# Experts with one token tile and the third token tile: the up product with tokens stationary and weights moving; attention scores in 64x64 array tiles; the last wait on SyncE

## What is computed

```python
# attention, per batch and head
y[t] = r[t] @ (state + outer(u * k[t], v[t]))
state = w[:, None] * state + outer(k[t], v[t])
# dense network, 384 -> 2048 -> 384
h = x @ w_in;  g = maximum(h, 0) + alpha * minimum(h, 0);  x = g @ w_out
# experts, 384 -> 1024 -> 384, at most 384 rows each, in order of the rows
e = argmax(x @ w_gate);  p = softmax(x @ w_gate)[e]
out[i] = p * (maximum(disp[e] @ w1[e], 0) @ w2[e])[pos[i]]   # 0 for rows over capacity
```

## Time and profile before

| | |
|---|---|
| median of 3 runs | 455.86 us (455.79 to 456.08) |
| the profiled execution | 453.51 us |
| its span, first to last instruction | 451.8 us |
| PE busy | 425.0 us (94%) |
| DVE, ACT, POOL busy | 257.5, 197.8, 175.9 us |
| granted clock of PE over the span | 0.981 |
| expert stage | 291.8 to 443.0 us |

### The profile page before, as it was taken

The page is one execution under the profiler, slowest core; times in us unless marked ns, Lnnn a source line. Parts: engine busy times, 40 slices in busy tenths (PEclk is TensorE's granted clock), DMA queues, the critical chain, the costliest instruction groups (busy, mean ns, idle before and its releaser), DMA issues.

```text
span 451.8 us, 8997 instructions
## 1 busy us (share of the span) xinstructions
PE 425.0 (94%) x3141; PEld 410.1 (91%) x3141; DVE 257.5 (57%) x555; ACT 197.8 (44%) x450; POOL 175.9 (39%) x189
## 2 busy tenths in 40 slices
PE   6799999999999999999999986899999999998892
PEld 5688889999999999999999985699999999998891
DVE  6688876766435343543437563444659574658730
ACT  2689944341311113111323332334668575558640
POOL 4999525554323523244435861511120210012102
PEclk9899999999999999999999997999999999999996
DMA  7996024437950100000012440684676875563000
GB/s 253 399 326 200 3 83 154 154 100 261 371 201 0 54 1 0 0 28 24 0 35 81 142 145 17 215 316 123 206 237 184 245 209 176 161 209 89 11 19 7
DMA packets 33935, 61.43 MB, mean 136 GB/s; under 512 B 4655, under 2 KB 26911, under 8 KB 33889
## 3 DMA queue, kind: packets, MB, share of 16 engines
q1 hardware_dynamic: 31008, 55.53, 37.7%
q0 software_dynamic: 2880, 5.29, 3.5%
HBM read 47.53 MB, written 14.79 MB: 138 GB/s over the span
## 4 chain that ended last, share of the span: by engine, by line
PE 80%; DVE 7%; ACT 5%; issue 3%; POOL 2%; DMA 0%; POOLq 0%; ACTq 0%; DVEq 0%
PE bank L1146 20%; PE bank L1161 19%; PE bank L1271 16%; PE bank L1300 14%; ACT scores L610 2%; PE bank L1052 2%; PE bank L1079 2%; PE bank L1115 2%; ACT w_high L595 1%; PE bank L1107 1%; PE bank L1258 1%; PE bank L1067 1%; DVE neg L883 1%; DVE act_full L889 1%; DVE xe_low L1002 1%
## 5 line engine op out<-in xcount | busy, mean ns | idle before, releaser
L509 POOL TENSOR_TENSOR g_low<-act_full,g_high 128x384 fp32r<-128x384 f32 x63 | 63.7, 1010 | 115.2 <-ACT g_high L641 115.2
L641 ACT ACTIVATE g_high<-act_full 128x384 fp32r<-128x384 f32 x64 | 33.7, 526 | 150.0 <-DVE act_full L889 137.4
L1146 PE MATMUL bank<-x_split,w_high 128*128 (+1 forms) x384 | 98.4, 337 | 0.0
L883 DVE TENSOR_SCALAR neg<-bank,alpha_sb 128x384 f32<-128x384 f32 x64 | 39.2, 613 | 71.6 <-PE bank L1146 71.5
L565 POOL DMA_INDIRECT out<-y_out,token x24 | 24.8, 1032 | 125.2 <-ACT y_out L728 124.3
L1146 PEld LDWEIGHTS bank<-x_split,w_high 128*128 128x128 f32 x384 | 69.0, 188 | 0.2 <-issue 0.2
L1161 PE MATMUL bank<-w_high,g_high 128*128 128x384 f32 x189 | 65.1, 344 | 1.2 <-POOL g_low L509 1.2
L1146 PE MATMUL bank<-x_split,w_low 128*128 (+1 forms) x192 | 64.4, 336 | 0.0
L1161 PE MATMUL bank<-w_high,g_low 128*128 128x384 f32 x189 | 63.8, 338 | 0.0
L1161 PE MATMUL bank<-w_low,g_high 128*128 128x384 f32 x189 | 63.8, 337 | 0.0
L1271 PE MATMUL bank<-xe_high,w_high 128*128 128x256 f32 (+1 forms) x192 | 58.0, 302 | 1.7 <-DVE xe_low L1002 1.7
(11 more groups left out here) (127 smaller groups left out, 800.7 us busy)
## 6 DMA issues: line engine op xcount, KB each, us to landing
w_raw<-chunks SPq DMA_DIRECT2D x96, 192.0 KB, 3.2
w_raw<-chunks SPq DMA_DIRECT2D x32, 384.0 KB, 3.1
rk_in<-att_rk SPq DMA_DIRECT2D x12, 704.0 KB, 6.5
routed_rows<-fill SPq DMA_DIRECT2D x1, 5211.0 KB, 17.7
xe<-routed_rows SPq DMA_DIRECT2D x7, 579.0 KB, 5.3
v_in<-att_v SPq DMA_DIRECT2D x12, 200.0 KB, 5.2
out<-fill SPq DMA_DIRECT2D x1, 2304.0 KB, 22.9
x_split<-x_split POOLq DMA_DIRECT2D x18, 48.0 KB, 2.5
```

Source lines behind the costliest of these rows:

```text
L509: pool.tensor_tensor(gl[:, f % 4, :], act_full[:, f % 2, :], gh[:, f % 4, :].bitcast(f32), ALU.subtract).then_inc(s_gl, 1)
L641: act.activation(gh[:, f % 4, :], act_full[:, f % 2, :], ACT.Copy).then_inc(s_gh, 1)
L883: dve.tensor_scalar(neg[:, f % 2, :], h, 0.0, alpha_sb[:, f:f + 1], ALU.min, ALU.mult)\
L1146: last = mm(bank[f % 4][:, 0:G], a[:, f, w], x[:, kc, bass.ds(g * G, G)], start=kc == 0 and i == 0, stop=kc == KC - 1 and i == 2)
```

## The change

1. **One-tile experts** (`rows < P + 1`): the up product is turned round. `flip_up` holds a 128x128 block of tokens stationary and moves the w1 of four chunks, 512 columns, so 9 matmuls make half of the hidden layer, in a bank, with tokens on the partitions. DVE takes the relu into `gn` (`flip_relu`), PE transposes it in eight 128x128 pieces (`flip_turn`), ACT and DVE make the high and low parts (`flip_high`, `flip_low`), and `expert_down` goes on as before. The next expert's tokens are turned between the halves.
2. **Three-tile experts**: tiles 0 and 1 as before with 256 columns, the third by the same flipped way, its transposes in the middle of the first down product. The down products go 1, 2, 0 and so do the copies and scatters (`Y_ORDER`).
3. ACT's `flip_high(e, 2)` and DVE's `flip_relu(e, 2, ..)` and `flip_low(e, 2, ..)` run for every expert, also where there is no third tile; PE raises their semaphores (`s_fh[1]` before the down products, `s_ft[1]` after the first of two, or after five of eight chunks where there is one). PE's next use of banks 0 to 3 waits for them (`flip_banks_free`).
4. The low part of w1 (`split_low1`) moves from DVE to POOL, ahead of the expert's scatters.
5. **Scores** in four array tiles: two matmuls of 64 stationary columns in place of one of 128.
6. ACT in attention: diagonals, kn copy, y copy, with the y copy of the same step; kn copies wait for ruk, ruk no longer for kn copies, `k_turn` for both.
7. SP takes over the wait for the last scatter.

```diff
             sp.wait_ge(s_out, 16 * GT * (E - 1))
+            sp.wait_ge(s_last, 16 * GT)
...
-            for e in range(1, E):
-                for i in reversed(range(GT)):
-                    y_scatter(e - 1, i)
-
-                pool.wait_ge(s_out, e * 16 * GT)
-                pool.sem_inc(s_gone, 1)
-            for i in reversed(range(GT)):
-                y_scatter(E - 1, i, s_last)
-
-            pool.wait_ge(s_last, GT * 16)
+            def split_low1(e, f):
...
+            for e in range(E):
+                if e + FIRST < E:
+                    for f in range(NFE):
+                        split_low1(e + FIRST, f)
+                for i in Y_ORDER:
+                    y_scatter(e, i, s_out if e < E - 1 else s_last)
+                if e < E - 1:
+                    pool.wait_ge(s_out, (e + 1) * 16 * GT)
+                    pool.sem_inc(s_gone, 1)
...
             def kn_copy(t):
                 act.wait_ge(s_kt, t + 1)
+                if t:
+                    act.wait_ge(s_ruk, t + 1)
...
             for t in range(T):
-                if t:
-                    x_high(t - 1)
+                if t + 1 < T:
+                    diagonals(t + 1)
                 if t + 2 < T:
                     kn_copy(t + 2)
-                if t + 1 < T:
-                    diagonals(t + 1)
+                x_high(t)
                 if CT <= t < CT + EARLY:
                     split_high(t - CT)
-            x_high(T - 1)
...
+            def flip_high(e, i):
+                act.wait_ge(s_step, e * NFE + FFN_STEPS)
+                for half in range(2):
+                    act.wait_ge(s_ft[i // 2], 2 * e + half + 1)
+                    act.activation(egh[:, half * HF:(half + 1) * HF, i * P:(i + 1) * P],
+                                   bank[2 + half][:, :].rearrange("p (f n) -> p f n", f=HF), ACT.Copy)\
+                       .then_inc(s_fc[i // 2], 1)
+            for e in range(E):
+                with act.If(rows[e] < P + 1):
+                    if e < E - 1:
+                        for i in range(GT):
+                            xe_high(e + 1, i, bank[4 + GT - 1 - i])
+                    flip_high(e, 0)
                     if FIRST <= e + 1 < E:
-                        split_high2(e + 1, f)
-
-            for e in range(E):
-                with act.If(rows[e] < 2 * P + 1):
-                    ups(e, 2 * P)
+                        for f in range(NFE):
+                            split_high2(e + 1, f)
+                    act.sem_inc(s_mgh, NFE)
...
+                flip_high(e, 2)
                 for f in range(NFE):
                     if e + FIRST < E:
                         split_high1(e + FIRST, f)
                     if f in (3, 5, 7):
-                        y_copy(e, (7 - f) // 2)
+                        y_copy(e, Y_ORDER[(f - 3) // 2])
...
-                dve.wait_ge(s_kn, t + 1)
+                if t < 2:
+                    dve.wait_ge(s_kn, t + 1)
+                dve.wait_ge(s_kt, t + 1)
...
+            def flip_relu(e, i, half):
+                dve.wait_ge(s_fh[i // 2], 2 * e + half + 1)
+                if i:
+                    dve.wait_ge(s_ft[0], 2 * e + 2)
+                elif e:
+                    dve.wait_ge(s_ft[1], 2 * e)
+                dve.tensor_scalar(gn[:, half * HF * P:(half + 1) * HF * P], bank[half][:, :], 0.0, None, ALU.max)\
+                   .then_inc(s_fr[i // 2], 1)
+            def flip_low(e, i, half):
+                dve.wait_ge(s_fc[i // 2], 2 * e + half + 1)
...
+                if i:
+                    op.then_inc(s_fl, 1)
+                else:
+                    op.then_inc(s_mgl, HF)
+            for e in range(E):
+                with dve.If(rows[e] < P + 1):
+                    flip_relu(e, 0, 0)
+                    if e < E - 1:
+                        for i in range(GT):
+                            xe_low(e + 1, i, bank[4 + GT - 1 - i])
+                    flip_relu(e, 0, 1)
+                    for half in range(2):
+                        flip_low(e, 0, half)
                     if FIRST <= e + 1 < E:
-                        split_low2(e + 1, f)
-
-            for e in range(E):
-                with dve.If(rows[e] < 2 * P + 1):
-                    ups(e, 2 * P)
+                        for f in range(NFE):
+                            split_low2(e + 1, f)
...
+                for half in range(2):
+                    flip_relu(e, 2, half)
+                for half in range(2):
+                    flip_low(e, 2, half)
                 if e < E - 1:
                     keep_meta(e + 1)
-                if e + FIRST < E:
-                    for f in range(NFE):
-                        split_low1(e + FIRST, f)
...
+                reuse(pe, s_kn, t)
...
-                    for h2 in range(2):
-                        p = slice(h2 * HALF, (h2 + 1) * HALF)
-                        last = mm(a_bank(t, h2)[:, a * P:(a + 1) * P], k_hat[p, t % 3, a, :],
-                                  r_hat[p, t % RH, a, :], start=True, stop=True)
+                    for half in range(2):
+                        for h2 in range(2):
+                            p = slice(h2 * HALF, (h2 + 1) * HALF)
+                            tokens = slice(half * HALF, (half + 1) * HALF)
+                            last = mm(a_bank(t, h2)[tokens, a * P:(a + 1) * P], k_hat[p, t % 3, a, tokens],
+                                      r_hat[p, t % RH, a, :], start=True, stop=True)
...
+            def flip_banks_free(e, b):
+                if b < 2:
+                    pe.wait_ge(s_fr[1], 2 * (e - 1) + 1 + b)
+                else:
+                    pe.wait_ge(s_fl, 2 * (e - 1) + b - 1)
...
+            def flip_up(e, i, half):
+                slot = e * NFE % SLOTS + half * HF
+                w1_ready(pe, e, half * HF + HF - 1)
                 if i:
-                    last.then_inc(s_yd[i], 1)
+                    pe.wait_ge(s_mgl, e * NFE + HF + half + 1 + C_MGL)
+                elif e:
+                    pe.wait_ge(s_mgl, (e - 1) * NFE + HF + half + 1 + C_MGL)
+                    flip_banks_free(e, half)
+                for kc in range(KC):
+                    for m, (x, w) in enumerate(((xeh, wh), (xeh, wl), (xel, wh))):
+                        last = mm(bank[half][:, :].rearrange("p (f n) -> p f n", f=HF),
+                                  x[:, e % 2, kc, i * P:(i + 1) * P], w[:, slot:slot + HF, kc * P:(kc + 1) * P],
+                                  start=kc == 0 and m == 0, stop=kc == KC - 1 and m == 2)
+                last.then_inc(s_fh[i // 2], 1)
+            def flip_turn(e, i):
+                for half in range(2):
+                    pe.wait_ge(s_fr[i // 2], 2 * e + half + 1)
+                    if i:
+                        pe.wait_ge(s_mgl, e * NFE + NFE + C_MGL)
+                    elif e:
+                        pe.wait_ge(s_mgl, e * NFE + C_MGL)
+                        flip_banks_free(e, 2 + half)
+                    for k in range(HF):
+                        f = half * HF + k
+                        last = pe.transpose(bank[2 + half][:, k * P:(k + 1) * P], gn[:, f * P:(f + 1) * P], ident[:, :])
+                    last.then_inc(s_ft[i // 2], 1)
...
-                with pe.If(rows[e] < 2 * P + 1):
-                    expert_ups(e, 2 * P)
-                    turned(e, 2)
-                    pe.sem_inc(s_yd[2], 1)
+                with pe.If(rows[e] < P + 1):
+                    pe.sem_inc(s_mh, NFE)
+                    flip_up(e, 0, 0)
+                    if e < E - 1:
+                        for i in range(GT):
+                            if e:
+                                y_bank_free(e, GT - 1 - i)
+                            turn_xe(e + 1, i, bank[4 + GT - 1 - i])
+                    flip_up(e, 0, 1)
+                    pe.sem_inc(s_w1free, 1)
+                    flip_turn(e, 0)
+                    pe.sem_inc(s_fh[1], 2)
+                    no_tile(e, 1)
+                    no_tile(e, 2)
+                    expert_down(e, 0, range(HF + 1))
+                    pe.sem_inc(s_ft[1], 2)
+                    expert_down(e, 0, range(HF + 1, NFE))
                 with pe.Else():
-                    expert_ups(e, CAP)
-                    expert_down(e, 2)
-                with pe.If(rows[e] < P + 1):
-                    turned(e, 1)
-                    pe.sem_inc(s_yd[1], 1)
-                with pe.Else():
-                    expert_down(e, 1)
-                expert_down(e, 0)
+                    pe.sem_inc(s_fh[0], 2)
+                    pe.sem_inc(s_ft[0], 2)
+                    with pe.If(rows[e] < 2 * P + 1):
+                        expert_ups(e, 2 * P)
+                        pe.sem_inc(s_w1free, 1)
+                        pe.sem_inc(s_fh[1], 2)
+                        no_tile(e, 2)
+                        expert_down(e, 1)
+                        pe.sem_inc(s_ft[1], 2)
+                        expert_down(e, 0)
+                    with pe.Else():
```

(9 more changed lines are left out.)

78 lines of the change are left out of this document (52 added, 26 removed).

## The result

| | before | after |
|---|---|---|
| median of the runs, us | 455.83 | 472.72 (471.53 to 475.67) |
| ratio | | 1.0388, 95% interval 1.0332 to 1.0445 |
| profiled execution, us (span) | 453.51 (451.8) | 473.54 (471.8) |
| granted clock, mean | 0.981 | 0.968 |
| ahead of and in the eight experts, us | 152.98 | 175.16 |

What follows compares the result with a forecast made beforehand. PE was taken to bound the kernel, with 80% of the chain that ended last. Terms -6.2 + 2.2 - 1.6 - 1.5 = -7.1 took the median from 455.86 to 448.8 us; range 445.0 to 453.5.

Steps and rivals of the forecast that it cites:

- Two-tile experts: PE has the same list: Experts with two token tiles: PE's work unchanged, costed at nothing; up to 1 us in each of three if cover is gone.
- Prices: PE's time per matmul or transpose: 119.7 ns at 256 columns, 173.3 at 384, 227 estimated at 512, 110 per transpose.
- Rival 4: Wide matmuls on PE much cheaper, 130 ns at 512 columns, saving a further 8.7 us: 440 us; chance 3%.
- One-tile experts: Experts 5, 6 and 7 with the flipped up product: -6.2 us together, bounds -10 and -3.
- the empty passes: ACT's and DVE's unneeded third-tile work: 1.3 us at the start of experts 6 and 7 each, 1.2 once for late y copies.
- Three-tile experts: Experts 0 and 4: same columns plus new transposes on PE, +1.1 us each, +2.2 in all.
- Scores: Recurrence at the program's head, scores in 64x64 tiles: 0.18 us saved in each of ten steps, -1.6 us, bounds 0 and -2.5.
- rival 3: Recurrence: only two of the four score tiles run side by side, giving 457.2 us, slower; chance 7%.
- Last wait: Program's end: with the wait on SP, POOL's drain starts earlier, -1.5 us, bounds 0 and -1.65.
- Rival 2: Program's end: the drain ends when it did, everything else as forecast: 450.3 us; chance 13%.
- Rival 1: Experts: helper engines slower than costed, through contention between DVE's and POOL's splits plus longer waits: 451.5 us; chance 17%.
- rival 1 with the drain unmoved: Upper end of the range: slower helper engines in the experts and no gain at the program's end, put at 453.5 us.

Runs made afterwards that it cites:

- run 1: Kernel before, with a never-entered block of 360 PE instructions put ahead of each of the eight experts: 475.29 us, ratio 1.0401.
- run 2: Kernel before, with a never-entered block of 60 PE instructions put ahead of each of the eight experts: 455.55 us, ratio 1.0021.
- run 3: Changed kernel with PE's expert code written as short conditional blocks, shared work standing once, other engines' programs unchanged: 447.39 us, ratio 0.9844 to before.
- run 8: Changed kernel in short blocks, with ACT's and DVE's third-tile passes run only in three-tile experts: 445.14 us, ratio 0.9774 to before.
- run 9: Changed kernel in short blocks, with the split of the first weight halves moved back from POOL to DVE: 448.61 us, ratio 0.9839 to before.
- run 5: Kernel before, with one jumped-over block of 130 PE instructions ahead of the experts, so their code stands later: 452.83 us, ratio 0.9946.
- run 6: Kernel before, with never-entered blocks of 600, 40, 440, 120, 360, 200, 520 and 280 PE instructions ahead of experts 0 to 7: 479.29 us, one execution.
- run 10: Changed kernel in short blocks, but three-tile experts with the old 384-column up products and no third-tile passes on any engine: 462.59 us, ratio 1.0154 to before.

## Why the prediction was wrong

- **The step that failed: "Two-tile experts: PE has the same list", costed at nothing.** PE has the same matmuls, but it reaches them by other jumps. I counted instructions that run, not those that are jumped over, and so had no term for the branches of any expert. That term was +26 us (the changed kernel against the same in short blocks, runs 1 to 3), more than all the others together, and lay outside the range. No rival held it, and the chance of "slower" was laid on the score tiles, with a sliver for the helpers.
- **By parts**, changed kernel against before, profiled executions: the start -1.45 us (the first dense product starts at 60.40, before 61.84), the end -1.2 (the last matmul to the end of the span), the middle +0.5, the experts 175.16 - 152.98 = +22.2; together +20.0, as the two times differ. In the experts: standstills ahead of experts 0, 2, 3 and 4 and inside expert 2, about 20 us more than before (8.25 - 1.97, and 2.07, 2.76, 4.51 and 4.95), clock about 6.7 (36 matmuls each of experts 0, 3 and 4 in 6.40, 5.87 and 5.88, and 24 of expert 2 in 4.4, against 4.31 and 2.9).
- **Prices were right.** Flipped matmuls of 512 columns start every 230 ns (227 said, an estimate), from the timeline of expert 5:

```profile
426.06 0.40 PE L1401 MATMUL bank<-w_high,xe_low 128*128 128x512 f32 x1
426.29 0.39 PE L1401 MATMUL bank<-w_high,xe_high 128*128 128x512 f32 x1
426.52 0.39 PE L1401 MATMUL bank<-w_low,xe_high 128*128 128x512 f32 x1
```

  Rival 4 falls with them, and the figure of about 131 ns of the Trainium skill (TensorE: Matmul & The Clock Gate, Back-to-back issue gap) is not what this kernel shows.
- **One-tile experts**, -6.2 said: in short blocks 37.4 us against 43.2, -5.8. That is partly luck, since two parts were off and against each other. PE idles 1.0 us, not 0.5, for the low half ahead of the down product (3.1 us in three), but the empty passes cost 0.9 us in all (run 8), not 3.8.
- **Three-tile experts**, +1.1 each said: expert 4 takes 27.12 against 25.97, +1.15. Expert 0 shows it where the clock was the same (27.1 in run 8, 26.1 before).
- **Scores**, -1.6 said, -1.45 found. Four tiles do run side by side, so rival 3 falls. PE's timeline of one step of after (start to start 0.93, before 1.09):

```profile
50.91 1.10 PE L1138 MATMUL bank<-r_hat,k_hat 64*64 64x128 f32 x32
51.84 1.05 PE L1166 MATMUL bank<-r_hat,state 64*64 64x128 f32 x16
```

- **Last wait**, -1.5 said: from the last store's end (467.04 after, 445.45 before) to the drain's end it is 4.5 us, before 6.1: -1.6. Rival 2 falls. The drain itself got longer (4.475 us before) and starts ahead of the store's end, where the prediction kept its length and moved its start:

```profile
L161 POOLq DRAIN  x1: 6047/6047/6047, 465.5 to 465.5; - x1
```

- The sum of my terms was -7.1. The changed kernel in short blocks gives -7.2 against its own before. That is partly luck: 2 of it come from the old code's place in its packets, and the clock took 1.5 back in that profile.
- **Rival 1**, slower helpers (451.5 us), has no sign in runs 3 and 9: 447.39 and 448.61 us.
- **Slips in the prediction**, none of which decides: the change touches PE's work in five experts, not three; 0.18 us in ten steps are 1.8, not 1.9; its terms give expert 5 12.8 us, not 12.6; rival 1 with the drain unmoved is 453.0, not 453.5; and the chances add up to 101%.

## What to carry to other kernels

Before adding a case to a branch, list how many instructions each case jumps over on the engine that bounds the kernel, and look at the duration of its branch records as at any other line. Share the work of the cases, and put only the difference under a condition. Here a never-entered block of up to 200 instructions took 0.2 to 0.4 us by itself, one of 360 and more 1.4 to 6.4, but for one whose price fell on the next branch. Between these, and where short jumps follow one another, it depends on the place: jumps over 163 and 211 took 0.2 to 0.4 us in most cases and up to 4.0 in some, with no long jump near. In run 3's profile, too, three branches took 1.0 to 1.8 us, beside queued matmuls. So a kernel in short blocks has to be measured as well, and its branch records read again after each change. Where a change to one part moves the time of another whose code is the same, look at where that code now stands.

## What the runs showed of the hardware

- Blocks of code that a kernel never enters cost 20 us at 360 instructions each (run 1) and nothing clear of noise at 60 (run 2); code shifted by 130 instructions gained 2 (run 5).
- PE also stands in straight code behind jumps, until the next packet has come: 2.5 us at expert 2 of the changed kernel. A short jump behind a long one took 5.67 us (run 6), one of 49 behind one of 163 3.65 (run 10).
- A standstill of 8.25, 4.5 or 4.95 us is followed by matmuls at the lower clock each time, one of 2.1 us sometimes: the same code of PE at 0.60 in one profile (run 3) and 1.00 in another (run 8).
- What stays open: what sets the time within a length (440 instructions took 5.31 and 3.66 us). The long ones came early, beside full DMA queues (share 1.06 ahead of expert 0), and still a jump took 4.4 us at the end of the changed kernel, where the page's last slice has 12 GB/s. A good part of the difference is how late the packet itself starts: in the changed kernel 3.5 us after the branch at expert 0, 0.4 to 1.7 us after the other eight long ones. No run separated load from place.
